# Edits to a fused attention and feed-forward kernel: prologue, last head, last tile

## The chip, the cores and the metric

The kernel runs on one core of a Trainium2 chip. The metric is the device time of one execution in microseconds. The kernel before takes 997.59 us (median of 3 runs, 997.53 to 998.23). The core has TensorE (matmul), VectorE, ScalarE and GpSimd, which run their own instruction streams and meet at semaphores, and SyncE, which issues most of the transfers.

## The reference

```python
# q, k, v: (2, 8, 768, 64), proj: (64, 6)
q_bits = (q @ proj > 0); k_bits = (k @ proj > 0)
mask = bucket(q_bits)[:, :, :, None] == bucket(k_bits)[:, :, None, :]
scores = where(mask, q @ k.T / 8, -1e9)
scores = scores - max(scores)
attn = exp(scores); attn = attn / (sum(attn) + 1e-9)
x = heads_side_by_side(attn @ v)                 # 1536 x 512
h = x @ w_in; x = (h - tanh(h)) @ w_out          # 512 -> 2048 -> 512
p = probs / (probs.sum(-1) + 1e-9)               # 4 experts
out = sum_e p[:, e] * (max(x @ w1[e], 0) @ w2[e])  # 512 -> 1024 -> 512
```

All is fp32 in and out. There are 16 heads (batch 2 by 8) of 768 tokens.

## The kernel before, in words

Matmuls are made in fp32r; where precision wants it, an operand is split into a rounded part (`hi`) and the rest (`lo`), and products of the parts are added in PSUM. The rounded parts are mostly made by ScalarE, the rests by VectorE or GpSimd.

**Attention.** Heads 0 to 15 are taken in pairs, in `pair(it)` on every engine; `b` is the head within the pair, `qt` the tile of 128 queries, `t` = 6b + qt. Per tile TensorE makes the scores (`score`, L1491, two tiles ahead of the rest), VectorE clamps them into `prob` with the row's extreme (`clamp`, L1097), ScalarE takes the exp (`take_exp`, L790), TensorE turns the six 128x128 blocks (`turn`, L1524), ScalarE rounds them out of PSUM (`round_turned`, L797) and VectorE takes the rest (`rest_turned`, L1104). From these, `weigh` (L1543) multiplies by v: the first half of a head's queries while its own tiles 4 and 5 run, the second half during tiles 1 to 3 of the next head. The results stand in `o_ps` and are moved out by ScalarE (`move_o`, L805); `weigh` waits for that move. Head 15 has no next head: its first half is moved by `move_last` and summed by VectorE (`last_sum`, L1215), its second half is made inside the first block of the feed-forward part (`finish_attention`).

**Masks.** The bits of q and k are made by four matmuls per half of the tokens (`bits`, L1480) with the projection matrix, and thresholded. They write to half of a score slot, the side slot. For head 0 the matrix has to be loaded and split first, on VectorE (L1078 to L1090).

**Inverse sums.** ScalarE's exp gives row sums; GpSimd adds eps, VectorE takes the reciprocal (`invert`, L1158), TensorE turns it (`turn_inverse`, L1489) into the side slot, VectorE copies it out (`take_inverse`, L1163), SyncE stores it to DRAM and spreads it back over 64 partitions (`spread_inverse`), and GpSimd multiplies (`x_scale`). For the last pair VectorE multiplies (`last_scale`, L1223).

**Slots.** Two PSUM slots take the scores in turn (`slot_of`). In the middle of each head one turn is left out, as the side slot is in use: the score of tile 3 goes where that of tile 2 was and waits for that tile's clamp.

**Feed-forward.** Hidden groups of 256 run in blocks of 384 tokens (`place_block`): seven products (L1596) per block by a scheme that needs sums and differences of quarters, with the down products (L1619, L1627) of the block before between them. The second part ends with six down tiles of 128 tokens by 512 columns, each added to the output by VectorE (L1299) and stored by its own DMA (L465).

The order of work on each engine is that of the code, written out by hand. A wait stands in the stream of its engine, and everything behind it on that engine waits too.

Around the change, before:

```python
for _ in range(6):                                   # TensorE, L1578: warm-up
    pe.matmul(o_ps[:, 0:HALF], x_f32[:, 0:P], x_f32[:, 0:HALF], start=True, stop=True)
...
elif qt == SIDE + first + 1 and not first:           # score: tile 4
    pe.wait_ge(inv_turn_taken, h)
```

## Time and profile before

| | |
|---|---|
| median of 3 runs | 997.59 us |
| the profiled execution | 997.7 us |
| its span, first to last instruction | 995.9 us |
| TensorE busy | 984.6 us (99%) |
| VectorE busy | 672.7 us (68%) |
| ScalarE busy | 463.3 us (47%) |
| GpSimd busy | 450.7 us (45%) |
| attention ends, first block begins | 234.20 us |

Times in the rows are microseconds from the start of the span. PE is TensorE's matmul, PEld its weight load, DVE VectorE, ACT ScalarE, POOL GpSimd, SP SyncE. L numbers are lines of the kernel before. Ends of matmuls are modelled, and a busy TensorE is not one at its peak.

### The profile page before, as it was taken

The numbers are of one execution on the slowest core, as the hardware profiler recorded it, in microseconds if no ns is written. First come the engines' busy times: TensorE is split into PE (matmuls) and PEld (weight loads), VectorE is DVE, ScalarE is ACT, GpSimd is POOL, SyncE is SP. The second block draws the span as 40 slices with busy tenths as digits, with TensorE's granted clock in tenths as the row PEclk, the third lists the DMA queues.
The fourth block names the chain that finished last, engine by engine and source line by source line (L and its number), as shares of the span: only waits on it lengthen the run. The fifth ranks groups of instructions, "written<-read, shape, count | busy, mean of one in ns | idle before, by whom it ended". The sixth has DMA issues, their size and how long they took to land.

```text
span 995.9 us, 16472 instructions
## 1 busy us (share of the span) xinstructions
PE 984.6 (99%) x5406; PEld 910.0 (91%) x5406; DVE 672.7 (68%) x1121; ACT 463.3 (47%) x853; POOL 450.7 (45%) x440
## 2 busy tenths in 40 slices
PE   7999999999999999999999999999999999999998
PEld 5999999988999999999988898989989899888997
DVE  7988888887856465565996556565565655656555
ACT  6888788887544443444542323223232232322321
POOL 6578779998664473644634304123041230412100
PEclk9999999999999999999999999999999999999999
DMA  5576656661101001010020100201002010020002
GB/s 144 160 179 178 164 161 174 170 172 36 61 22 44 22 21 63 21 42 21 22 64 22 43 22 21 63 21 42 21 21 63 21 42 21 21 64 21 21 24 102
DMA packets 50789, 65.20 MB, mean 65 GB/s; under 512 B 5345, under 2 KB 32449, under 8 KB 50753
## 3 DMA queue, kind: packets, MB, share of 16 engines
q1 hardware_dynamic: 50448, 64.48, 22.9%
q10 hardware_dynamic: 240, 0.30, 0.1%
q8 instruction: 15, 0.25, 0.1%
q14 instruction: 22, 0.17, 0.1%
q0 software_dynamic: 64, 0.00, 0.0%
HBM read 43.87 MB, written 3.19 MB: 47 GB/s over the span
## 4 chain that ended last, share of the span: by engine, by line
PE 92%; DVE 4%; POOL 1%; ACT 1%; issue 1%; DMA 0%; DVEq 0%; ACTq 0%; POOLq 0%
PE ps L1596 33%; PE ps L1619 26%; PE ps L1627 12%; PE ps L1543 7%; PE ps L1513 6%; PE ps L1524 6%; PE ps L1480 2%; DVE xq_raw L1136 1%; DVE hb L1268 1%; POOL wu_lo L622 0%; POOL g_lo L699 0%; DVE xq_lo L1148 0%; ACT wu_hi L834 0%; DVE pT_lo L1104 0%; ACT prob L790 0%
## 5 line engine op out<-in xcount | busy, mean ns | idle before, releaser
L1596 PE MATMUL ps<-xq_hi,wu_lo 128*128 128x384 f32 x672 | 227.1, 338 | 0.7 <-POOL wu_lo L622 0.4
L1596 PE MATMUL ps<-xq_hi,wu_hi 128*128 128x384 f32 x672 | 226.2, 337 | 0.0
L1596 PE MATMUL ps<-xq_lo,wu_hi 128*128 128x384 f32 x672 | 226.0, 336 | 0.0
L622 POOL TENSOR_TENSOR wu_lo<-wu_raw,wu_hi 128x768 fp32r<-128x768 f32 (+1 forms) x48 | 104.8, 2203 | 221.4 <-ACT wu_hi L834 221.3
L1299 DVE SCALAR_TENSOR_TENSOR acc<-ps,p_norm,acc 128x512 f32<-128x512 f32 x180 | 135.0, 750 | 100.9 <-PE ps L1619 95.3
L1619 PE MATMUL ps<-wd_lo,g_hi 128*128 128x512 f32 x384 | 150.9, 393 | 0.0
L1619 PE MATMUL ps<-wd_hi,g_hi 128*128 128x512 f32 x384 | 150.9, 393 | 0.0
L1619 PE MATMUL ps<-wd_hi,g_lo 128*128 128x512 f32 x384 | 150.6, 392 | 0.0
L1596 PEld LDWEIGHTS ps<-xq_hi,wu_lo 128*128 128x128 f32 x672 | 126.1, 188 | 6.6 <-DVE hb L1257 0.9
L1596 PEld LDWEIGHTS ps<-xq_lo,wu_hi 128*128 128x128 f32 x672 | 126.2, 188 | 3.8
L1596 PEld LDWEIGHTS ps<-xq_hi,wu_hi 128*128 128x128 f32 x672 | 126.1, 188 | 0.0
L989 ACT ACTIVATE g_hi<-hb 128x384 fp32r<-128x384 f32 x96 | 50.3, 525 | 161.8 <-DVE hb L1257 96.1
L699 POOL TENSOR_TENSOR g_lo<-hb,g_hi 128x384 fp32r<-128x384 f32 x64 | 72.8, 1138 | 104.5 <-ACT g_hi L912 104.5
L1104 DVE TENSOR_TENSOR pT_lo<-ps,pT_hi 128x512 fp32r<-128x512 f32 x144 | 94.7, 685 | 17.6 <-ACT pT_hi L797 17.2
L790 ACT ACTIVATE prob<-prob,neg_max 128x768 f32<-128x768 f32 x96 | 90.2, 939 | 29.2 <-DVE prob L1097 28.1
L1097 DVE TENSOR_SCALAR_CACHE_REDUCE prob<-ps 128x768 f32<-128x768 f32 x96 | 90.7, 946 | 2.9 <-PE ps L1513 2.8
L1619 PEld LDWEIGHTS ps<-wd_hi,g_hi 128*128 128x128 f32 x384 | 72.1, 188 | 16.7
L1627 PE MATMUL ps<-g_hi,wd_lo 128*128 128x384 f32 x256 | 86.1, 336 | 1.2 <-POOL g_lo L699 0.8
L1627 PE MATMUL ps<-g_hi,wd_hi 128*128 128x384 f32 x256 | 86.1, 336 | 0.0
L1627 PE MATMUL ps<-g_lo,wd_hi 128*128 128x384 f32 x256 | 85.9, 336 | 0.0
L797 ACT ACTIVATE pT_hi<-ps 128x512 fp32r<-128x512 f32 x144 | 80.3, 592 | 9.0 <-PE ps L1524 8.2
L1619 PEld LDWEIGHTS ps<-wd_hi,g_lo 128*128 128x128 f32 x384 | 72.1, 188 | 12.5
(130 smaller groups left out, 1760.7 us busy)
## 6 DMA issues: line engine op xcount, KB each, us to landing
wu_raw<-in_w SPq DMA_DIRECT2D x64, 128.0 KB, 2.8
wd_raw<-in_w SPq DMA_DIRECT2D x16, 512.0 KB, 3.3
q_raw<-in_qT SPq DMA_DIRECT2D x28, 192.0 KB, 3.2
k_raw<-in_kT SPq DMA_DIRECT2D x28, 192.0 KB, 3.3
wu_raw<-in_w_in SPq DMA_DIRECT2D x32, 128.0 KB, 2.6
wd_raw<-in_w_out SPq DMA_DIRECT2D x8, 512.0 KB, 3.5
v_raw<-in_vP SPq DMA_DIRECT2D x16, 192.0 KB, 2.8
inv_rows<-inv_dram SPq DMA_DIRECT2D x16, 192.0 KB, 3.2
```

Of the source, the lines that this page charges most:

```text
L622: rest = pool.tensor_tensor(wu[par][1][:, slots, :, :], wu_raw[:, slots, :, :], wu[par][0][:, slots, :, :].bitcast(F32), ALU.subtract)
L699: pool.tensor_tensor(g_lo[par][:, f, l * HALF:(l + 1) * HALF], hb[:, h, :], g_hi[par][:, f, l * HALF:(l + 1) * HALF].bitcast(F32), ALU.sub ...
L790: act.activation(prob[t % 3][:], prob[t % 3][:], ACT.Exp, bias=neg_max[:, t:t + 1], scale=-1.0, accum_out=total[:, t:t + 1]).then_inc(exp_ ...
L797: act.activation(pT_hi_flat[:, m * BANK:(m + 1) * BANK], turn_ps[m % 3], ACT.Copy).then_inc(pT_hi_ready, 1)
L1097: dve.tensor_scalar(prob[t % 3][:], score_ps[slot][:, 0:S], MASKED, None, ALU.min, ALU.min, accum_out=neg_max[:, t:t + 1]).then_inc(clampe ...
L1104: dve.tensor_tensor(pT_lo_flat[:, cols], turn_ps[m % 3], pT_hi_flat[:, cols].bitcast(F32), ALU.subtract).then_inc(pT_lo_ready, 1)
L1299: dve.scalar_tensor_tensor(out=part_of, in0=source, scalar=scale, in1=part_of, op0=ALU.mult, op1=ALU.add).then_inc(down_taken, 1)
L1513: mm = pe.matmul(score_ps[slot_of(b, qt, first)][:, k0:k1], x[:, rows], y[:, k0:k1], start=m == 0, stop=m == 1)
L1543: mm = pe.matmul(o_ps[:, 0:HALF].rearrange("p (t c) -> p t c", c=P), v_st[b][:, k, :], x[:, n * HT:(n + 1) * HT, k, :], start=first, stop= ...
L1596: mm = pe.matmul(to, w[:, wslot, k, :], x[:, xslot, k, :], start=start and k + m == 0, stop=k == 1 and m == 2, skip_group_check=not start)
L1619: mm = pe.matmul(to, x[:, f, rows], y[:, f, :], start=f + m == 0, stop=f == FC - 1 and m == 2)
L1627: mm = pe.matmul(to, x[:, f, rows], y[:, f, cols], start=f + m == 0, stop=f == FC - 1 and m == 2)
```

## The change

**Prologue.** The two `lo` halves of head 0's k go from GpSimd to VectorE. VectorE makes the first `lo` half of q before the projection matrix is there. The warm-up has five matmuls in place of six. **Last head.** For head 15 the score slots alternate without the turn left out; the score of tile 3 moves ahead of the weights at tile 1; the turned inverse of head 14 is no longer taken there. ScalarE's move of head 14's first half stands ahead of an exp; the move of its second half goes to VectorE. GpSimd's `x_add` stands behind `v_round` and `v_rest`. VectorE's rests of the last tile stand ahead of the reciprocal and `last_sum(0)`. **Inverses.** Those of heads 14 and 15 are turned by one transpose behind the third product of the first block and copied together; SyncE stores and spreads both. **Last tile.** The last down tile is made, added and stored as two halves of 256 columns.

```diff
-        def slot_of(b, qt, first):
-            return ((QT + 1) * b + qt + (qt >= SIDE + first)) % 2
+        def slot_of(b, qt, first, ends=False):
+            return ((QT + 1) * b + qt + (qt >= SIDE + first and not ends)) % 2
@@ SyncE
+                def spread_last():
+                    sp.wait_ge(inv_turn_taken, HEADS - 1)
+                    for b in range(2):
+                        store_inverse(HEADS - 2 + b, b)
+                    sp.wait_ge(inv_stored, 16 * HEADS)
+                    sp.wait_ge(x_ready, PAIRS - 1)
+                    for b in range(2):
+                        spread_rows(HEADS - 2 + b, b)
...
-                for k, t in enumerate(tiles_of(True)):
+                for k, t in enumerate(tiles_of(True)[:-1]):
...
+                for n in range(2):
+                    sp.wait_ge(down_taken, first_tile(I2, 0, True) + n)
+                    sp.dma_start(out[start:start + P, n * SPLIT:(n + 1) * SPLIT],
+                                 acc2[:, at + n * SPLIT:at + (n + 1) * SPLIT]).then_inc(stored, 16)
@@ GpSimd
-                            if later and b == 1:
+                            if later and b == 1 and not last:
                                 x_add(it - 1)
                         if qt == 1:
                             v_round(h, b)
                             v_rest(h, b)
+                            if last and b == 1:
+                                x_add(it - 1)
...
-                for n in range(2):
...
-                    pool.tensor_tensor(k_st[0][D:P, tokens(n)], k_raw[D:P, tokens(n)],
-                                       k_st[0][D:P, tokens(n)].bitcast(F32),
-                                       ALU.subtract).then_inc(k0_lo_ready if n == 0 else k_lo_ready, 1)
@@ ScalarE
-                        if qt == 3 and last and b == 1:
-                            move_o(h - 1, 1 - b, 1, it)
+                        if qt == 0 and last and b == 1:
+                            move_o(h - 1, 1 - b, 0, it)
                         if not (last and t == TILES - 1):
                             take_exp(i + 1, (t + 1) % TILES)
-                        if qt == 0 and not first:
+                        if qt == 0 and not first and not (last and b == 1):
@@ VectorE
+                first_q_rest(0)
                 dve.wait_ge(p_loaded, 32)
...
-                            if not first:
+                            if not first and more:
                                 take_inverse(h - 1, 1 - b, side_slot(b, first))
...
+                        if qt == 3 and last and b == 1:
+                            move_second(h - 1, 1 - b)
...
+                first_k_rest(0)
+                first_q_rest(1)
+                first_k_rest(1)
...
-                invert(HEADS - 1, 1)
...
+                rest_turned(HEADS - 1, QT - 1)
+                invert(HEADS - 1, 1)
                 last_sum(0)
-                rest_turned(HEADS - 1, QT - 1)
...
-                    if start:
-                        take_inverse(HEADS - 1, 1, slots[1])
                     first()
+                    if start:
+                        take_last_inverses()
@@ TensorE
-                    if qt == SIDE + first:
+                    if is_last(h):
+                        pe.wait_ge(clamped, i - 1)
+                    elif qt == SIDE + first:
                         pe.wait_ge(clamped, i)
...
-                        if qt != 1 + first and not (first and qt == 4):
+                        if (qt != 1 + first and not (first and qt == 4)) or not more:
                             next_score()
...
-                        if qt == 1 and not more:
-                            turn_inverse(h - 1, side_slot(b, first))
...
-                for _ in range(6):
+                for _ in range(5):
...
                 def finish_attention(part):
-                    if part == 0:
-                        turn_inverse(HEADS - 1, slots[1])
+                    if part == 1:
+                        turn_inverse(HEADS - 1, slots[0])
                     weigh(HEADS - 1, 1, 1, part)
-                    if part == 0:
-                        pe.wait_ge(inv_turn_taken, HEADS)
...
+                pe.wait_ge(inv_turn_taken, HEADS - 1)
                 place_block(0, 1, False, between=last_output)
...
+                for n in range(2):
+                    cols = slice(n * SPLIT, (n + 1) * SPLIT)
+                    pe.wait_ge(down_taken, first_tile(I2, 0, True) + n - 4)
+                    for f in range(FC):
+                        for m, (x, y) in enumerate(((h, wl), (l_, wh), (h, wh))):
+                            mm = pe.matmul(d_ps[(n + 3) % 4][:, 0:SPLIT], x[:, f, rows], y[:, f, cols],
+                                           start=f + m == 0, stop=f == FC - 1 and m == 2)
+                    mm.then_inc(down_full, 1)
```

How the change moves instructions shows in three places. The first is VectorE in the prologue, from the scalings of the projection matrix on. Before:

```order
L1078 TENSOR_SCALAR proj_f32<-proj_raw 128x6 [waits const_ready,p_loaded]
L1078 TENSOR_SCALAR proj_f32<-proj_raw 128x6 x3
L1082 CAST projq_h0<-proj_f32 64x64 [waits proj_ready]
...
L1090 TENSOR_TENSOR projq_hl<-proj_f32,projq_hl 64x64
L1190 SCALAR_TENSOR_TENSOR q_lo0<-q_raw,q_hi0 64x384 [waits q0_hi_first]
L1190 SCALAR_TENSOR_TENSOR q_lo0<-q_raw,q_hi0 64x384 [waits q_hi_ready]
L1195 TENSOR_SCALAR k_hi0<-ps,bit_from 64x384 [waits bits0_first]
```

And VectorE in the same place of the changed kernel:

```order
L1100 SCALAR_TENSOR_TENSOR q_lo0<-q_raw,q_hi0 64x384 [waits q0_hi_first]
L1114 TENSOR_SCALAR proj_f32<-proj_raw 128x6 [waits const_ready,p_loaded]
...
L1126 TENSOR_TENSOR projq_hl<-proj_f32,projq_hl 64x64
L1106 TENSOR_TENSOR k_st0<-k_raw,k_st0 64x384 [waits k0_hi_first]
L1100 SCALAR_TENSOR_TENSOR q_lo0<-q_raw,q_hi0 64x384 [waits q_hi_ready]
L1106 TENSOR_TENSOR k_st0<-k_raw,k_st0 64x384 [waits k_hi_ready]
L1236 TENSOR_SCALAR k_hi0<-ps,bit_from 64x384 [waits bits0_first]
```

One subtraction went ahead of the scalings, and two of k_st were added between the matrix and the first bits.

The second place is TensorE at tiles 0 and 1 of the last head, from the end of tile 0's turn on (prob0). Its weights for head 14 read pT and v_st0. Before:

```order
L1524 MATMUL ps<-ident,prob0 128x128
L1543 MATMUL ps<-pT_lo,v_st0 128x384 [waits o_moved,pT_lo_ready,v_lo_ready,clamped]
L1543 MATMUL ps<-pT_hi,v_st0 128x384
L1543 MATMUL ps<-pT_lo,v_st0 128x384
L1543 MATMUL ps<-pT_hi,v_st0 128x384
L1489 MATMUL ps<-ident,inverse 128x128 [waits inverted]
L1524 MATMUL ps<-ident,prob1 128x128 [waits exp_ready]
L1524 MATMUL ps<-ident,prob1 128x128
L1524 MATMUL ps<-ident,prob1 128x128 [waits pT_lo_ready]
L1524 MATMUL ps<-ident,prob1 128x128 x3
L1513 MATMUL ps<-k_hi1,q_lo1 128x512 [waits clamped]
```

And TensorE there in the changed kernel, where the four matmuls of L1569 are the score of tile 3:

```order
L1580 MATMUL ps<-ident,prob0 128x128
L1569 MATMUL ps<-k_hi1,q_lo1 128x512 [waits clamped]
L1569 MATMUL ps<-k_hi1,q_lo1 128x256
L1569 MATMUL ps<-k_st1,q_hi1 128x512
L1569 MATMUL ps<-k_st1,q_hi1 128x256
L1599 MATMUL ps<-pT_lo,v_st0 128x384 [waits pT_lo_ready,o_moved,v_lo_ready]
L1599 MATMUL ps<-pT_hi,v_st0 128x384
L1599 MATMUL ps<-pT_lo,v_st0 128x384
L1599 MATMUL ps<-pT_hi,v_st0 128x384
L1580 MATMUL ps<-ident,prob1 128x128 [waits exp_ready]
```

The score stands ahead of the weights, and the turn of the inverse is gone.

The third place is VectorE from the last head's last clamp (prob2) into the first block. Before:

```order
L1097 TENSOR_SCALAR prob2,neg_max<-ps 128x768 [waits score_full]
L1104 TENSOR_TENSOR pT_lo<-ps,pT_hi 128x512 [waits pT_hi_ready] x3
L1158 RECIPROCAL inverse<-total_eps 128x6 [waits eps_added]
L1215 TENSOR_TENSOR x_f32<-ps,pv_other 64x384 [waits x_ready,o_moved]
L1104 TENSOR_TENSOR pT_lo<-ps,pT_hi 128x512 [waits pT_hi_ready] x2
L1163 COPY inv_turned<-ps 6x128 [waits inv_turn_full]
L1247 TENSOR_TENSOR hb<-ps,hb 128x384 [waits c1_ready,sum11_full]
L1268 TENSOR_TENSOR hb<-hb,tanh_h0 128x384 [waits tanh_ready]
```

And VectorE there in the changed kernel, with the added move of o_ps (pv0) as the first row:

```order
L1204 COPY pv0<-ps 128x384 [waits o_full]
L1133 TENSOR_SCALAR prob2,neg_max<-ps 128x768 [waits score_full]
L1140 TENSOR_TENSOR pT_lo<-ps,pT_hi 128x512 [waits pT_hi_ready] x5
L1194 RECIPROCAL inverse<-total_eps 128x6 [waits eps_added]
L1255 TENSOR_TENSOR x_f32<-ps,pv_other 64x384 [waits x_ready,o_moved]
L1293 TENSOR_TENSOR hb<-ps,hb 128x384 [waits c1_ready,sum11_full]
L1272 COPY inv_turned<-ps 38x128 [waits inv_turn_full]
L1314 TENSOR_TENSOR hb<-hb,tanh_h0 128x384 [waits tanh_ready]
```

The sum over o_ps (x_f32) moved behind the last two rests of pT, and the copy of the inverses behind the block's first sum.

## Rows read from the trace of the kernel before

**Rows 1.** Page, section 1: busy us (share of the span) xinstructions

```profile
PE 984.6 (99%) x5406; PEld 910.0 (91%) x5406; DVE 672.7 (68%) x1121; ACT 463.3 (47%) x853; POOL 450.7 (45%) x440
```

**Rows 2.** Busy time by stretch: us; PE, PEld, DVE, ACT, POOL; PEclk, DMA, GB/s

```profile
0.00:24.00 24.00, 18.98 (x88) 13.98 (x89) 18.30 (x46) 15.38 (x29) 14.67 (x28) 1.00 0.55 142
...
248.30:985.00 736.70, 735.67 (x3844) 685.62 (x3845) 454.46 (x695) 261.57 (x454) 251.98 (x203) 1.00 0.11 35
```

**Rows 3.** Timeline, prologue: start, us, engine, line, operation [idle before <-releaser]

```profile
5.57 1.00 POOL L676 TENSOR_TENSOR k_st<-k_raw,k_st 64x384 fp32r<-64x384 f32 x1 [1.88 <-ACT k_st L773]
5.65 0.97 DVE L1082 CAST projq_h<-proj_f 64x64 fp32r<-64x64 f32 x1
...
6.86 0.22 DVE L1086 TENSOR_TENSOR projk_ll<-proj_f,projk_hh 128x64 fp32r<-128x64 f32 x1
...
7.01 1.00 POOL L676 TENSOR_TENSOR k_st<-k_raw,k_st 64x384 fp32r<-64x384 f32 x1 [0.44 <-ACT k_st L773]
7.09 0.99 DVE L1088 TENSOR_TENSOR projq_h<-proj_f,projk_hh 64x64 fp32r<-64x64 f32 x1
...
8.26 1.02 DVE L1190 SCALAR_TENSOR_TENSOR q_lo<-q_raw,q_hi 64x384 fp32r<-64x384 f32 x2
...
9.07 0.41 PE L1480 MATMUL ps<-q_lo,projq_h 128*128 128x384 f32 x1 [1.36 <-DVE q_lo L1190]
```

**Rows 4.** Timeline, ScalarE in the prologue

```profile
3.94 0.53 ACT L770 ACTIVATE q_hi<-q_raw 64x384 fp32r<-64x384 f32 x1
```

**Rows 5.** Timeline, TensorE's weight loads in the warm-up

```profile
5.35 0.34 PEld L1579 LDWEIGHTS ps<-x_f 128*128 128x128 f32 x1 [0.30 <-issue]
...
5.94 1.16 PEld L1579 LDWEIGHTS ps<-x_f 128*128 128x128 f32 x4 [0.25 <-issue]
```

**Rows 6.** Timeline, last head

```profile
222.93 0.49 ACT L805 ACTIVATE pv<-ps 128x384 f32<-128x384 f32 x1
...
223.67 0.41 PE L1543 MATMUL ps<-pT_lo,v_st 128*128 128x384 f32 x1 [0.82 <-ACT pv L805]
...
224.96 0.67 DVE L1104 TENSOR_TENSOR pT_lo<-ps,pT_hi 128x512 fp32r<-128x512 f32 x1
...
229.67 0.95 DVE L1097 TENSOR_SCALAR_CACHE_REDUCE prob<-ps 128x768 f32<-128x768 f32 x1
...
232.29 0.44 PE L1524 MATMUL ps<-ident,prob 128*128 128x128 f32 x2 [0.36 <-DVE pT_lo L1104]
```

**Rows 7.** Chain of work that ended last, one score: start us, us, what

```profile
216.55 0.70 PE ps L1513 x4
```

**Rows 8.** Timeline, end of the last head and first block; page, section 6

```profile
234.20 0.42 PE L1596 MATMUL ps<-xq_hi,wu_lo 128*128 128x384 f32 x1
...
234.34 0.56 DVE L1215 TENSOR_TENSOR x_f<-ps,pv_other 64x384 f32<-64x384 f32 x1
...
234.96 1.29 DVE L1104 TENSOR_TENSOR pT_lo<-ps,pT_hi 128x512 fp32r<-128x512 f32 x2
...
236.40 0.42 PE L1543 MATMUL ps<-pT_lo,v_st 128*128 128x384 f32 x1
...
247.17 1.82 DVE L1223 TENSOR_TENSOR acc<-x_f,inv_rows 128x384 f32<-128x384 f32 x2
...
248.25 0.41 PE L1627 MATMUL ps<-g_hi,wd_lo 128*128 128x384 f32 x1 [0.83 <-POOL g_lo L699]
...
inv_rows<-inv_dram SPq DMA_DIRECT2D x16, 192.0 KB, 3.2
```

**Rows 9.** The end: chain, timeline, and busy time of one stretch

```profile
984.46 8.22 PE ps L1619 x36
...
992.70 0.75 DVE L1299 SCALAR_TENSOR_TENSOR acc<-ps,p_norm,acc 128x512 f32<-128x512 f32 x1 [0.61 <-PE ps L1619]
993.47 0.33 SPq L465 DMA_DIRECT2D out<-acc  x1
...
994.25:995.05 0.80, 0.00 (x0) 0.00 (x0) 0.00 (x0) 0.00 (x0) 0.00 (x0) 1.00 0.87 328
```

More of the change, by code:

```diff
@@ L1074, in _, with first_q_rest, first_k_rest @@
                 dve.memset(projq_h0[D:P, qs].bitcast(F32), 0.0)
+                def first_q_rest(n):
+                    dve.wait_ge(q0_hi_first if n == 0 else q_hi_ready, 1)
+                    dve.scalar_tensor_tensor(out=q_lo[0][0:D, tokens(n)], in0=q_raw[0:D, tokens(n)], scalar=QSCALE,
+                                             in1=q_hi[0][0:D, tokens(n)].bitcast(F32), op0=ALU.mult,
+                                             op1=ALU.subtract).then_inc(q0_lo_first if n == 0 else q_lo_ready, 1)
+                def first_k_rest(n):
+                    dve.wait_ge(k0_hi_first if n == 0 else k_hi_ready, 1)
+                    dve.tensor_tensor(k_st[0][D:P, tokens(n)], k_raw[D:P, tokens(n)],
+                                      k_st[0][D:P, tokens(n)].bitcast(F32),
+                                      ALU.subtract).then_inc(k0_lo_ready if n == 0 else k_lo_ready, 1)
+                first_q_rest(0)
                 dve.wait_ge(p_loaded, 32)
@@ L1171, in pair @@
                             ahead = (t + 1) % TILES
-                            clamp(i + 1, ahead, slot_of(ahead // QT, ahead % QT, first and qt < QT - 1))
+                            clamp(i + 1, ahead, slot_of(ahead // QT, ahead % QT, first and qt < QT - 1,
+                                                        is_last(2 * it + ahead // QT) and t < TILES - 1))
                         if first and qt == 2:
@@ L1185, in pair @@
                             invert(h - 1, 1 - b)
-                for n in range(2):
-                    dve.wait_ge(q0_hi_first if n == 0 else q_hi_ready, 1)
-                    dve.scalar_tensor_tensor(out=q_lo[0][0:D, tokens(n)], in0=q_raw[0:D, tokens(n)], scalar=QSCALE,
-                                             in1=q_hi[0][0:D, tokens(n)].bitcast(F32), op0=ALU.mult,
-                                             op1=ALU.subtract).then_inc(q0_lo_first if n == 0 else q_lo_ready, 1)
+                        if qt == 3 and last and b == 1:
[3 more added lines that the diff above has]
+                first_k_rest(1)
                 def first_bits(n, to, own, done):
@@ L1512, in score @@
                         for k0, k1 in ((0, BANK), (BANK, S)):
-                            mm = pe.matmul(score_ps[slot_of(b, qt, first)][:, k0:k1], x[:, rows], y[:, k0:k1],
+                            mm = pe.matmul(score_ps[slot_of(b, qt, first, is_last(h))][:, k0:k1], x[:, rows], y[:, k0:k1],
                                            start=m == 0, stop=m == 1)
@@ L1711, in _ @@
                         place_block(i, r, True)
-                for k in range(BT):
+                for k in range(BT - 1):
                     down_tile(I2 - 1, 3, True, k)
+                (wh, wl), h, l_ = wd[1], g_hi[1], g_lo[1]
+                rows = slice(tiles_of(True)[BT - 1] * P, (tiles_of(True)[BT - 1] + 1) * P)
+                for n in range(2):
+                    cols = slice(n * SPLIT, (n + 1) * SPLIT)
[5 more added lines that the diff above has]
+                    mm.then_inc(down_full, 1)
 def kernel(**inputs):
```

55 lines of the change are left out of this document (38 added, 17 removed).

## The prediction

> **What bounds the kernel now.** I read the busy shares first: TensorE is busy 984.6 of the span's 995.9 us [rows 1]. Then the stretches: from 248.3 to 985 us TensorE is busy 735.67 of 736.70 us, in the first 24 only 18.98 [rows 2]. So nothing off TensorE's path counts in the long middle, and whatever time a start gains there is carried to the end undiminished. The change lives where TensorE waits: the prologue, the last head with the first block behind it, and the tail after the last matmul. The timeline of each says what it waits for. The profiled execution took 997.7 us, 1.8 more than its span; the median of the runs is 997.59, so I make the sum against 997.7 and take 0.1 off. What a measurement can tell from no change is 0.2%, 2.0 us: faster means below 995.6.
>
> **Prologue.** The first projection matmul starts at 9.07, when VectorE has run a chain that began with the projection matrix's arrival and ends with q_lo [rows 3]. Two links stand out. A cast of 64x64 starts at 5.65 and takes 0.97 us; a subtraction of 64x64 starts at 7.09 and takes 0.99. A subtraction of 128x64, with GpSimd quiet, takes 0.22. GpSimd's two k_st subtractions run at 5.57 to 6.57 and 7.01 to 8.01, and the slow VectorE instructions end 0.05 and 0.07 after them. The change takes these two off GpSimd. If the long durations are the wait for GpSimd, 0.97-0.22 = 0.75 and 0.99-0.22 = 0.77, 1.52 together, go; if they belong to the 64x64 forms themselves, nothing goes. No row has such a form with GpSimd quiet, so the bounds are 0 and 1.6; I take 1.5, since both ends fit GpSimd's.
> The Trainium skill (SBUF — State Buffer, Who interferes with whom) says the pair of ports that VectorE shares with GpSimd is locked for a whole instruction, and that casts and instructions with two SBUF inputs can be held. By it the gain is the full 1.5; with long forms as the cause it would be 0. The trace agrees in both ends.
>
> What VectorE gets in return: the first q_lo half goes ahead of the matrix (ScalarE's q_hi starts at 3.94 and takes 0.53 [rows 4]; 0.51 long by the pair's 1.02, it is over by 5.0, and the cast's own inputs, four small scalings of the matrix, are made right before 5.65), so it costs nothing. In its old place stands one k_st half of the same size, again about 0.5 (between 0.5, the pair's half, and GpSimd's 1.00). The first group of four matmuls thus starts at about 9.07-1.5 = 7.55. The second group now needs a q_lo half and a k_st half more: VectorE ends them 1.0 after the first, about 8.3, and TensorE would reach them four matmuls (of 0.175 each: twelve such take 2.1 in the first block [rows 8]) after 7.55, at 8.25. At most 0.2 is lost, and VectorE's own next work, the first bits, waits only for the first group. ScalarE's part is not touched and runs ahead of its readers. GpSimd's later steps (the scaling of head 1) wait for ScalarE, not for the removed work, so they stay where they are; their cover is the first scores and exps that TensorE has to get through before head 1's bits. Warm-up: one matmul of six goes, 0.58 us at the quick pace; six end at some 7.4 and would just stand in front of a start at 7.5. Term: **-1.5**, bounds 0 and -1.6.
>
> The warm-up's weight load at 5.35 takes 0.34 after 0.30 of idleness, 0.64 in all; from 5.94 four come in 1.16 us [rows 5]. TensorE then rests until 9.07 and still works at the quick pace. In the changed kernel it works 0.6 us less and rests less. The granted clock of the stretch is 1.00, the 2.4 GHz level [rows 2]. I see no reason for a slow start, and keep it as a rival.
> The Trainium skill (TensorE: Matmul & The Clock Gate, What's actually happening) says that the clock rises by TensorE having been busy and falls by idleness. It speaks against a shorter warm-up; by it the start could be slow, which is rival 4. The trace has the quick pace before the last four loads, two of which stay.
>
> **Last head.** Before, TensorE stands 0.82 us until 223.67, waiting for ScalarE's move of o_ps that starts at 222.93; VectorE's first rest of head 15 stands until 224.96 behind the copy of the turned inverse, though its input is there at 223.9 [rows 6]. (Times between the rows shown are read from the same timeline.) Now score 9 needs an older clamp (slots alternate), stands ahead of the weights, and fills that hole: it costs the 0.70 that four score matmuls take [rows 7] but runs at 222.7 to 223.4; the move stands before an exp and is done at 222.5. The weights then go at 223.4 and the turn at 224.1 (224.55 before). VectorE rests tile 6 at 223.95 and clamps tile 9 at 224.6. Not all of that lasts: ScalarE's row of exp, round, x_round is full until 225.6 in both kernels, so the rests of tile 7 end at 227.5. Clamp 10 follows at 227.5, a rest at 228.4, then the added move on VectorE (0.56 like the 64x384 sum of rows 8), which puts clamp 11 at 229.65, where it was (229.67). What improves is behind it: ScalarE, rid of a move (0.49 in rows 6) and with its exp 10 from 228.4, rounds tile 9 by 230.4 instead of 231.9, so VectorE's rests start at 230.55 instead of 231.55. TensorE starts head 15's weights at 229.75 (230.21) and the second part of turn 10, which waited for VectorE until 232.29, at 231.25. From there on the work is the same, and the first block, at 234.20 before [rows 8], starts near 233.15: **-1.05**. Bounds: 0, if the added move makes VectorE the bound, and -1.5, the 1.0 of that rest and the move's 0.49.
>
> Queued behind what is moved: on GpSimd, x_add now comes after v_round and v_rest, which had waited behind it for a DMA; they come earlier and x_add no later. On SyncE, the two inverse rows of head 14 go to the end with those of head 15. Both are issued at about 238, spread at 241 and have landed at 244 (3.2 us each); their reader, last_scale, starts at 247.17, less some 0.6 [rows 8]. It is covered by 2 us and more; were it not, last_scale would hold VectorE and with it the second block.
>
> **First block.** Here the change costs. Before, the sum over o_ps runs at 234.34, in the hole before the last rests, which run from 234.96 to 236.25; weights start at 236.40, when TensorE's first twelve products end [rows 8]. Now the sum and a reciprocal (0.1) stand behind the rests, and the weights wait for the sum: 236.25+0.1+0.56 = 236.9, plus 0.05, against 236.4. That is 0.55 to 0.65 later, measured from the block's start. The inverse's turn leaves this place for one behind the third product, 0.1 each way. The copy of both inverses holds VectorE in order until that turn, so the first tanh subtraction starts some 0.7 later, but its reader on TensorE comes 8 us on. A part is given back: TensorE waited 0.83 us at 248.25 for GpSimd's g_lo, a chain that starts with ScalarE and GpSimd steps which keep their early time; the wait for it shrinks by 0.1 to 0.5. Net of the block: **+0.45**, bounds +0.1 and +0.7.
>
> **End.** The last tile takes six matmuls of 512 columns; VectorE's 0.75 at 992.70 follows; the store's issue at 993.47; its data move in one burst from 994.25 to 995.05 [rows 9]. Halved: twelve of 256 columns. Scores hold two of 512 and two of 256 in 0.70 [rows 7], the wide ones 0.228 apart (36 in 8.22 us), so a narrow one costs 0.12, and twelve cost 1.44 against 1.37: +0.07. VectorE's last instruction is half as wide: between 0.38 (half) and 0.56 (384 columns); I take 0.40, -0.35. The last store carries half the bytes: its burst is 0.35 shorter at the same rate; rows of 1 KB instead of 2 may eat a part, and the first half's burst may queue behind the tile before. I take -0.2, bounds 0 and -0.35. Term: **-0.5**, bounds -0.2 and -0.65.
>
> **Sum.** -1.5-1.05+0.45-0.5 = -2.6; 997.7-2.6 = 995.1, and 0.1 off for the median: **995.0**.
>
> **Rivals.**
> 1. The last head gives nothing: VectorE, with a move more, bounds it, and the late sum eats the rest. For it: clamp 11 comes no earlier in my walk. Against: ScalarE is rid of the same work. -1.5-0.5, 995.6; or 995.8 with a loss of 0.2.
> 2. The prologue gives little: the 64x64 forms are long by themselves, or a k_st half on VectorE takes 1.0. For it: no row of the form alone. Against: both ends match. -0.3-0.6-0.5 = -1.4, 996.2.
> 3. All ends well: the rests come early enough for the late sum to be hidden, and the stall at 248.25 takes up the block's loss: -1.6-1.4-0.6, some 994.0.
> 4. Slower: TensorE's clock is at 1.2 GHz when the bits start, for want of the sixth warm-up matmul. The place is 7.5 us; it decides if the quick pace has not come or is lost by then. Of the 18.98 us that TensorE is busy in the first 24, some 11 lie behind that point, and would double until it rises; two thirds of that on the path is +7, so -2.6+7: 1002. Against it: the quick pace came at 5.94 [rows 5], before the last four loads.
>
> **How the numbers follow.** Forecast 0.57 (own range 994.5 to 995.5), rival 1 0.16, rival 2 0.13, rival 3 0.10, rival 4 0.04. Faster by over 0.2%: 0.54 of the forecast, 0.10 of rival 3, half of rival 1, none of rival 2: 0.71. Slower: rival 4, 0.04, and 0.01 for the rest. Same: 0.24. The range of 8 in 10 reaches from rival 3 to rival 2: 993.9 to 996.3.
>
> **What would show it.** In the profile of the changed kernel: the 64x64 cast and subtraction near 0.2 us and the first projection matmul near 7.5; no wait for ScalarE's move at the last head's second tile; the first block's first matmul 2.5 us earlier than 234.20; a wait of about 0.6 on the sum over o_ps ahead of the weights in it; last_scale not waiting for a DMA; a last VectorE instruction near 0.4. The prediction is wrong if the cast stays at 1 us, if TensorE's steps at 8 us are twice as long, or if the block starts less than 2 us earlier.

## The result and the profile after

The changed kernel takes **994.51 us** (median of 7 runs, 994.20 to 994.84) against 997.59 (7 runs); the ratio is 0.9967, 95% interval [0.9955, 0.9978]. The profiled execution has a span of 992.7 us against 995.9. So 3.2 us are gone in the profile, 3.1 in the medians; 2.6 were forecast. The busy shares of the page barely move:

```profile
PE 984.2 (99%) x5409; PEld 909.9 (92%) x5409; DVE 672.5 (68%) x1124; ACT 462.4 (47%) x852; POOL 447.9 (45%) x438
```

By stretch (columns as in [rows 2]), the first 24 us hold 1.36 us more of TensorE's work than before, and the stretch from 248.30 on holds the same 735.67:

```profile
0.00:24.00 24.00, 20.34 (x98) 15.30 (x99) 19.20 (x51) 16.25 (x30) 14.51 (x27) 1.00 0.58 149
...
248.30:985.00 736.70, 735.67 (x3841) 685.18 (x3840) 454.95 (x693) 258.93 (x450) 251.52 (x203) 1.00 0.11 34
```

The prologue's timeline, which answers to [rows 3]:

```profile
4.48 0.55 DVE L1100 SCALAR_TENSOR_TENSOR q_lo<-q_raw,q_hi 64x384 fp32r<-64x384 f32 x1 [1.36 <-ACT q_hi L792]
...
5.00 0.39 DVE L1114 TENSOR_SCALAR proj_f<-proj_raw 128x6 f32<-128x6 f32 x4
...
5.42 0.19 DVE L1118 CAST projq_h<-proj_f 64x64 fp32r<-64x64 f32 x1
...
6.08 0.22 DVE L1124 TENSOR_TENSOR projq_h<-proj_f,projk_hh 64x64 fp32r<-64x64 f32 x1
...
6.36 0.56 DVE L1106 TENSOR_TENSOR k_st<-k_raw,k_st 64x384 fp32r<-64x384 f32 x1
...
7.06 0.41 PE L1534 MATMUL ps<-q_lo,projq_h 128*128 128x384 f32 x1 [0.16 <-DVE k_st L1106]
...
8.23 0.41 PE L1534 MATMUL ps<-q_lo,projq_h 128*128 128x384 f32 x1 [0.23 <-DVE k_st L1106]
```

The cast fell from 0.97 to 0.19, the subtraction from 0.99 to 0.22. The second group waits 0.23 for a k_st half. The first bits matmul moved from 9.07 to 7.06. 0.23 of that is a scaling of the projection matrix that begins earlier in this execution (at 5.00, at 5.23 in the kernel before): the matrix landed at most 2.9 us after its issue instead of 3.2, and the scalings stand right behind the query half, without a wait.

The last head and the first block, which answer to [rows 6] and [rows 8]:

```profile
231.32 0.42 PE L1650 MATMUL ps<-xq_hi,wu_lo 128*128 128x384 f32 x1
...
233.50 0.56 DVE L1255 TENSOR_TENSOR x_f<-ps,pv_other 64x384 f32<-64x384 f32 x1
...
234.16 0.41 PE L1599 MATMUL ps<-pT_lo,v_st 128*128 128x384 f32 x1 [0.51 <-DVE x_f L1255]
...
245.49 0.41 PE L1681 MATMUL ps<-g_hi,wd_lo 128*128 128x384 f32 x1 [0.21 <-POOL g_lo L721]
```

The block begins at 231.32 instead of 234.20. The weights wait 0.51 for the late sum, as foreseen, but the wait for g_lo shrinks from 0.83 to 0.21 and gives most of the loss back. VectorE's `last_scale` starts without a wait for a DMA, as foreseen too. The end, by the chain of work that ended last and the timeline ([rows 9]):

```profile
988.57 1.44 PE ps L1774 x12
...
990.04 0.48 DVE L1509 SCALAR_TENSOR_TENSOR acc<-ps,p_norm,acc 128x256 f32<-128x256 f32 x1 [0.23 <-PE ps L1774]
```

**Where the 3.2 us lie.** I cut the path at four marks that both kernels have: the first score, ScalarE's first round of the last head, the first matmul of the block, the matmul that waits for g_lo. The changed kernel was profiled a second time (label after_again below), with VectorE's first scaling of the projection matrix at 5.23 as before; that profile is the fair one to subtract. The scaling stands at 5.23 for another reason there: the matrix has landed (3.0 us after its issue, 3.2 in the kernel before), but the query half ahead of it runs from 4.75, as ScalarE's rounding of it came at 4.20 and not at 3.93. The first two marks in the timeline of the kernel before:

```profile
12.02 0.61 PE L1513 MATMUL ps<-k_hi,q_lo 128*128 128x512 f32 x2 [1.29 <-DVE k_hi L1195]
...
221.03 1.09 ACT L797 ACTIVATE pT_hi<-ps 128x512 fp32r<-128x512 f32 x2 [0.39 <-PE ps L1524]
```

and in the changed kernel's second profile:

```profile
10.30 0.61 PE L1569 MATMUL ps<-k_hi,q_lo 128*128 128x512 f32 x2 [0.90 <-DVE k_hi L1236]
...
219.42 1.09 ACT L819 ACTIVATE pT_hi<-ps 128x512 fp32r<-128x512 f32 x2 [0.36 <-PE ps L1580]
```

| stretch | before | changed, second profile | difference |
|---|---|---|---|
| start to first score | 12.02 | 10.30 | -1.72 |
| to the last head's first round | 209.01 | 209.12 | +0.11 |
| to the block's first matmul | 13.17 | 11.90 | -1.27 |
| to the matmul waiting for g_lo | 14.05 | 14.17 | +0.12 |
| to the span's end | 747.65 | 747.21 | -0.44 |

The second row lies between 208.8 and 209.7 over all the profiles, with the same instructions. Two places make most of its scatter. A bits matmul near 68 us stands for a transfer in score_back and whole_tile, and a score near 61.7 us comes late by 0.15 to 0.49 in eight of the thirteen profiles of the other kernels, in both of the changed kernel among them. In order, score_back, then the first and the second profile of the changed kernel, whose rows name no releaser, then probe_write, whose row names one:

```profile
68.72 0.44 PE L1534 MATMUL ps<-q_lo,projq_h 128*128 128x384 f32 x1 [0.34 <-DMA q_lo<-k_st]
61.62 0.30 PEld L1569 LDWEIGHTS ps<-k_hi,q_lo 128*128 128x128 f32 x2 [0.34 <-issue]
61.70 0.30 PEld L1569 LDWEIGHTS ps<-k_hi,q_lo 128*128 128x128 f32 x2 [0.21 <-issue]
62.51 0.61 PE L1576 MATMUL ps<-k_hi,q_lo 128*128 128x512 f32 x2 [0.26 <-DMA k_hi<-bits_kq]
```

The one profile of the kernel before has no such gap. So the +0.11 may be the landing of a transfer that differs from run to run, or a piece of the prologue's gain that is lost because TensorE now reaches this place earlier; one profile of the kernel before doesn't decide it. VectorE's first scaling also starts anywhere from 4.96 to 5.36. So below I read a small effect from the stretch in which the edit lies, and give the median beside it.

### The profile page after: what moved, and what is told of

Same layout as the page of the kernel before. It is cut to its first block, busy times and chain, and to the rows that moved or that the text cites. A ratio compares the mean times of both kernels' runs of the same rounds, so it can differ in the third digit from the quotient of the medians.

```text
span 992.7 us, 16478 instructions
## 1 busy us (share of the span) xinstructions
PE 984.2 (99%) x5409; PEld 909.9 (92%) x5409; DVE 672.5 (68%) x1124; ACT 462.4 (47%) x852; POOL 447.9 (45%) x438
## 4 chain that ended last, share of the span: by engine, by line
PE 92%; DVE 4%; ACT 1%; POOL 1%; issue 1%; DMA 0%; DVEq 0%; ACTq 0%; POOLq 0%
PE ps L1650 33%; PE ps L1673 26%; PE ps L1681 12%; PE ps L1599 7%; PE ps L1569 6%; PE ps L1580 6%; PE ps L1534 2%; DVE xq_raw L1172 1%; DVE hb L1314 1%; POOL wu_lo L651 0%; DVE pT_lo L1140 0%; POOL g_lo L721 0%; DVE xq_lo L1184 0%; ACT wu_hi L856 0%; ACT pT_hi L819 0%
```

## The experiments

All were run in three sets, each with the kernel before on the same chip (997.63 to 997.68). The changed kernel itself is in the third set only (994.28, where the first set of its runs gave 994.51), so a difference of 0.2 between medians of different sets says nothing.

**k_on_pool.** The key rests back on GpSimd; the early query half stays on VectorE.

```diff
-                first_k_rest(0)
-                first_k_rest(1)
+                pool.tensor_tensor(k_st[0][D:P, tokens(n)], k_raw[D:P, tokens(n)],
+                                   k_st[0][D:P, tokens(n)].bitcast(F32), ALU.subtract)
```

> The changed kernel with one part of the prologue undone: the two halves of the key rest (64x384) are again worked out by GpSimd; the early first query half on VectorE stays. Theory (what the prologue gained is that GpSimd no longer runs an operation with two SBUF inputs beside VectorE's 64x64 casts): the two casts go from 0.19 and 0.22 back to 0.97 and 0.99 us, the first bits matmul comes 1.0 to 1.6 us later than 7.06, and the kernel takes 995.5 to 996.0 against 994.5. Rival (the casts are quick because the query half was put ahead of them, or because 64x64 costs what it costs on a given day): casts stay near 0.2 us, first matmul within 0.2 of 7.06, time 994.5.

Measured: 995.44 (994.99 to 995.99), ratio 0.9978 [0.9969, 0.9987]. Timeline of its prologue:

```profile
5.71 1.00 POOL L707 TENSOR_TENSOR k_st<-k_raw,k_st 64x384 fp32r<-64x384 f32 x1 [2.02 <-ACT k_st L804]
5.79 0.96 DVE L1127 CAST projq_h<-proj_f 64x64 fp32r<-64x64 f32 x1
...
7.14 0.99 POOL L707 TENSOR_TENSOR k_st<-k_raw,k_st 64x384 fp32r<-64x384 f32 x1 [0.44 <-ACT k_st L804]
7.22 0.99 DVE L1133 TENSOR_TENSOR projq_h<-proj_f,projk_hh 64x64 fp32r<-64x64 f32 x1
```

The long forms are back at once, and the first bits matmul is 1.35 later (8.41); the time is just under the range expected. From the matrix's scaling to the first score it takes 6.02 us; the changed kernel takes 5.07, the kernel before 6.79. So of the prologue's 1.72 the key rests on VectorE are worth 0.95 once the query half is ahead, and the query half put ahead is worth 0.77. This is the swap that the prediction counted: the query half leaves the path, a key half of 0.56 takes its place, and the two instructions that GpSimd held give back 1.55.

**probe_read.** Nothing is undone; work that nobody reads is added on GpSimd.

```diff
+                pool.memset(acc[:, 6, :], 0.0)
+                # when the key halves are rounded, n = 0, 1:
+                pool.tensor_tensor(acc[D:P, 6, tokens(n)], acc[D:P, 6, tokens(n)], acc[D:P, 6, tokens(n)], ALU.add)
```

> The changed kernel with work added on GpSimd alone that nothing waits for: a clearing of a spare tile and, at the two moments at which the kernel before worked out the key rests, two additions of that tile to itself (64x384, two SBUF inputs). VectorE keeps all that the change gave it. Theory of the held port: though no data hangs on them, they bring the casts of 64x64 back to near 1 us, hold the rests on VectorE too, and put the first bits matmul 1.0 to 1.7 us later: 995.5 to 996.2. Rival (order on VectorE did it, GpSimd's work only mattered by its results): nothing moves, 994.5.

Measured: 995.86 (995.44 to 996.19), ratio 0.9983 [0.9974, 0.9992], 1.35 over the changed kernel's first median. Its timeline:

```profile
5.51 0.19 DVE L1125 CAST projq_h<-proj_f 64x64 fp32r<-64x64 f32 x1
5.58 0.82 POOL L707 TENSOR_TENSOR acc<-acc 64x384 f32<-64x384 f32 x1 [1.22 <-ACT k_st L802]
5.62 0.84 DVE L1126 CAST projk_hh<-proj_f 128x64 fp32r<-128x64 f32 x1
...
7.02 0.86 POOL L707 TENSOR_TENSOR acc<-acc 64x384 f32<-64x384 f32 x1 [0.61 <-ACT k_st L802]
...
7.11 1.19 DVE L1113 TENSOR_TENSOR k_st<-k_raw,k_st 64x384 fp32r<-64x384 f32 x1
```

The 64x64 cast, begun before GpSimd's addition, keeps its 0.19; the next one, of 128x64, is held until that addition ends (6.46 against 6.40). The subtraction of 64x384 is held too, 1.19 instead of 0.56, and ends 0.42 after the second addition. Shape is not the point; who is running is. The result of these additions is read by nobody, so GpSimd's running alone does it. This settles rival 2 of the prediction against it.

**probe_write.** The same two moments, with two clearings instead of two additions.

```diff
-                    pool.tensor_tensor(acc[D:P, 6, tokens(n)], acc[D:P, 6, tokens(n)], acc[D:P, 6, tokens(n)], ALU.add)
+                    pool.memset(acc[:, 6, :], 0.0)
```

> As the earlier run with two added GpSimd additions, but with two clearings (128x768, 0.73 us each) in their place, at the same moments. If any work of GpSimd on SBUF holds VectorE, the casts or rests beside it take 0.7 us longer and the first score comes 0.5 to 1.4 us later: 995.0 to 995.9. If only an operation that reads two SBUF operands does, nothing is held: 994.5 within 0.2.

Measured: 994.82 (994.35 to 995.40), ratio 0.9970 [0.9959, 0.9981]. The first score is at 10.89 against 10.30. Neither expectation holds whole:

```profile
5.25 0.94 DVE L1121 TENSOR_SCALAR proj_f<-proj_raw 128x6 f32<-128x6 f32 x4
5.39 0.77 POOL L707 MEMSET acc<- 128x768 f32 x1 [1.02 <-ACT k_st L802]
...
6.84 0.74 POOL L707 MEMSET acc<- 128x768 f32 x1 [0.68 <-ACT k_st L802]
6.90 0.22 DVE L1131 TENSOR_TENSOR projq_h<-proj_f,projk_hh 64x64 fp32r<-64x64 f32 x1
...
7.18 0.55 DVE L1113 TENSOR_TENSOR k_st<-k_raw,k_st 64x384 fp32r<-64x384 f32 x1
```

The first of these two clearings holds the four small scalings (0.94 instead of 0.37 to 0.39, their end 0.03 after its end); the second runs across three subtractions with two SBUF inputs and holds none (0.22 and 0.55, as with GpSimd quiet). The Trainium skill (SBUF — State Buffer, Who interferes with whom) draws this very line: an instruction with two SBUF inputs collides with GpSimd's reads and not with its writes, while casts and tensor-scalar forms can take the whole shared pair and collide with either. The rows agree for the subtractions and for the tensor-scalar form; a cast beside a clearing didn't come up here.

**warm0.** No warm-up matmul.

```diff
-                for _ in range(5):
+                for _ in range(0):
```

> The changed kernel without any of its five warm-up matmuls. If TensorE's clock is granted from the first real matmul on anyway, nothing moves (994.5, first quick pitch at once). If the clock stands at 1.2 GHz until TensorE has worked for a while, the bits, first scores and turns run at twice their time until it rises; the window from 7 to 12 us holds some 3 us of busy TensorE, so up to 2 to 3 us are lost there: 996 to 997.5. That prices the rival in which one warm-up fewer costs the clock.

Measured: 996.13, with times in two groups: 994.84 to 994.91 (3 runs) and 995.93 to 996.56 (8). The profile is of one in the first group (994.84). Its first bits matmuls are 0.32 us apart, where they are 0.17 apart with the warm-up, though the granted clock reads 1.00:

```profile
7.71 0.52 PE L1534 MATMUL ps<-q_hi,projq_hl 128*128 128x384 f32 x1
8.03 0.52 PE L1534 MATMUL ps<-k_st,projk_ll 128*128 128x384 f32 x1
...
11.34 0.51 PE L1569 MATMUL ps<-k_st,q_hi 128*128 128x512 f32 x2
```

By the first scores the pace is the quick one again. In this profile it costs 0.60 from the scaling to the first score (5.67 against 5.07). What the other eight runs lose beyond that, about 1.4 more (their median is 996.3), no profile shows; it stays open. The price of a slow start is thus some 0.6 to 2 us here, not the 7 of rival 4, and with five warm-ups it isn't paid at all: the bits matmuls of both profiles of the changed kernel are 0.17 apart.

**no_last_head.** Prologue and end as changed, last head and block as before (the two groups of edits taken into the kernel before).

> The kernel before with the prologue edits (early query half, key rests on VectorE, five warm-ups) and the halved last tile, but with the last head and the first block as they were. Theory by the traces: the prologue's -1.6 and the end's -0.5 stay, the last head's -1.27 and the block's +0.12 are gone, so +1.15 against the changed kernel: 995.6 (995.2 to 996.0). Rival (the prologue's gain is swallowed by the last head's wait for the spread rows if the head is left as it was): 996.5 or more.

Measured: 995.58 (995.25 to 996.28), ratio 0.9980 [0.9971, 0.9989]; expected 995.6. From the last head's first round to the g_lo matmul it takes 27.21 us, against 27.22 in the kernel before and 26.07 in the changed one: the last head and block are worth 1.14. It has the old waits, all of them:

```profile
221.60 0.41 PE L1561 MATMUL ps<-pT_lo,v_st 128*128 128x384 f32 x1 [0.82 <-ACT pv L804]
222.68 0.28 DVE L1175 COPY inv_turned<-ps 6x128 f32<-6x128 f32 x1 [0.86 <-PE ps L1507]
224.04 0.96 DVE L1109 TENSOR_SCALAR_CACHE_REDUCE prob<-ps 128x768 f32<-128x768 f32 x1 [0.48 <-PE ps L1531]
...
230.22 0.44 PE L1542 MATMUL ps<-ident,prob 128*128 128x128 f32 x2 [0.36 <-DVE pT_lo L1116]
```

**Three single undos in the last head.** move1_back puts the first move behind the exponential again, act_move the second move back on ScalarE, score_back the score of the second tile behind the weights and the turn.

```diff
move1_back
-                        if qt == 0 and last and b == 1:
-                            move_o(h - 1, 1 - b, 0, it)      # ahead of take_exp
-                        if qt == 0 and not first and not (last and b == 1):
+                        if qt == 0 and not first:            # behind take_exp
act_move
-                            move_second(h - 1, 1 - b)        # VectorE
+                            move_o(h - 1, 1 - b, 1, it)      # ScalarE
score_back
-                        if (qt != 1 + first and not (first and qt == 4)) or not more:
+                        if qt != 1 + first and not (first and qt == 4):
```

> The changed kernel with the first move of the last head behind the exponential on ScalarE again, as in the other heads. Theory A (the 0.82 us wait of the kernel before at the last head's first weights is that of this order alone): the first weights of the last head wait 0.6 to 0.8 us for pv, 0.5 to 0.8 us are lost: 995.0 to 995.3. Theory B (with the score issued a tile earlier, ScalarE's two operations stand before TensorE needs the bank, and the order is worth nothing): 994.5 within 0.15.

> The changed kernel with the second move of the last pair's values back on ScalarE, at its old place, instead of on VectorE. Theory A (ScalarE is the one that TensorE waits for in the last head, so 0.55 us more on it come back as waits for its rounds and exponentials): +0.3 to +0.6, 994.8 to 995.1. Theory B (the head was freed by the early first move and by the slots that alternate; the second move has slack on either engine): within 0.15 of 994.5.

> The changed kernel with the score that the last head issues at its second tile behind the weights and the turn again, as in the other heads; the score slots still alternate and nothing else is changed. Theory A (the score moved up is what keeps VectorE and ScalarE fed in the last head): TensorE waits 0.3 to 0.7 us more for the turned probabilities, 994.8 to 995.2. Theory B (only the order of equal work on TensorE, which has no wait there either way): within 0.15 of 994.5.

| | median | first round of the last head to g_lo matmul | against the changed kernel's 26.07 |
|---|---|---|---|
| move1_back | 994.41 | 26.10 | +0.03 |
| act_move | 995.05 | 26.56 | +0.49 |
| score_back | 994.61 | 26.18 | +0.11 |

move1_back has no wait for pv at all, and score_back lies within its theory B. act_move has the wait that theory A names; its chain starts at ScalarE, whose second move waits 0.78 for TensorE and pushes the next round:

```profile
226.85 0.49 ACT L827 ACTIVATE pv<-ps 128x384 f32<-128x384 f32 x1 [0.78 <-PE ps L1599]
...
228.16 1.07 ACT L819 ACTIVATE pT_hi<-ps 128x512 fp32r<-128x512 f32 x2
...
229.53 0.44 PE L1580 MATMUL ps<-ident,prob 128*128 128x128 f32 x2 [0.36 <-DVE pT_lo L1142]
```

score_back has a wait of 0.25 at its second tile, of which 0.11 is left later. The three sum to 0.63 of the 1.15 by which this stretch is shorter than before. The rest lies in what none of them undoes (the alternating slots, the inverse's turn and copy taken out of the head, GpSimd's and VectorE's new order), or in edits that cover for one another: move1_back may be worth nothing only because the score now stands ahead of the weights. Neither was tried, so how the last head's gain divides is in part open.

**sum_first and shift_halves.** Two attempts at a kernel that beats the changed one: the block's late sum put into VectorE's idle 1.02 us before 232.09; and on top of it the last pair's values shifted across the partitions in two halves.

```diff
+                last_sum(0)
                 rest_turned(HEADS - 1, QT - 1)
                 invert(HEADS - 1, 1)
-                last_sum(0)
```

```diff
-                            shift_part(h - 1, 1 - b, it)     # 2 transfers of 192 KB after the second move
+                            shift_halves(h - 1, it)          # 2 of 96 KB after each move
```

> The changed kernel with one thing moved on VectorE after the last head: the sum of the block's first half (x_f, 0.56 us) is put ahead of the last tile's rest and of the inverse of the last head, where VectorE idles 1.02 us before 232.09. Theory (the 0.51 us wait of TensorE at 234.16 for that sum is real and nothing later takes it up): the wait goes, the last weights come about 0.1 to 0.4 us sooner or, where the rest that is now behind the sum is late in its turn, nothing is gained: 994.1 to 994.4. Rival (the sum needs rows that land only at about 232, so VectorE now stands still before the rest and the weights for the rest come later than before): 994.6 to 995.2.

> The kernel with the sum put first (sum_first) and one thing more: the last pair's values are shifted across the partitions in two halves, each sent when its own half is moved, so that only half of the bytes leave at 227.9. In sum_first TensorE's wait at 234.16 is gone, but the one for g_lo at 245.5 grew from 0.21 to 0.74, and before it GpSimd works without a pause from 231.5, where it had waited 1.41 us for this transfer. Theory (GpSimd's chain from that landing sets the wait for g_lo): the landing is 0.4 to 0.7 earlier, the g_lo wait falls to 0.1 to 0.3, and the time is 0.3 to 0.6 under the changed kernel's: 993.9 to 994.3. Rival (the landing is by latency and not by bytes, or VectorE and the last sums hold the block): 994.5 as sum_first.

Measured: 994.58 (994.25 to 995.12) and 994.34 (994.11 to 995.03): no difference from 994.51 and 994.28, and less than either theory wanted. From the last head's first round to the g_lo matmul they take 25.97 and 25.95 against 26.07, 0.1 less. In sum_first the wait of 0.51 is gone, the block runs 0.5 ahead, and nearly all of it is waited away at one place, from 0.21 to 0.74:

```profile
231.54 0.56 DVE L1255 TENSOR_TENSOR x_f<-ps,pv_other 64x384 f32<-64x384 f32 x1 [0.41 <-ACT pv_other L834]
...
239.89 1.01 POOL L721 TENSOR_TENSOR g_lo<-hb,g_hi 128x384 fp32r<-128x384 f32 x1
240.09 1.23 DVE L1314 TENSOR_TENSOR hb<-hb,tanh_h 128x384 f32<-128x384 f32 x1
...
241.95 3.36 POOL L721 TENSOR_TENSOR g_lo<-hb,g_hi 128x384 fp32r<-128x384 f32 x2 [1.05 <-ACT g_hi L934]
...
242.41 2.04 DVE L1189 TENSOR_TENSOR wd_lo<-wd_raw,wd_hi 128x1024 fp32r<-128x1024 f32 x1
...
245.46 0.41 PE L1681 MATMUL ps<-g_hi,wd_lo 128*128 128x384 f32 x1 [0.74 <-POOL g_lo L721]
```

The hb subtraction has two SBUF inputs; it starts earlier than in the changed kernel (there 240.63, 0.61 us) and so falls longer under GpSimd's g_lo, and takes 1.23. It ends 0.42 after that g_lo, as the held 64x384 subtraction of probe_read did, and within 0.1 of its end in the changed kernel (241.24). In shift_halves the landing is 0.87 earlier (GpSimd starts at 230.65 instead of 231.52), more than I had expected, yet the wait for g_lo stays at 0.75 instead of falling, because GpSimd then waits for ScalarE:

```profile
230.65 1.82 POOL L590 TENSOR_TENSOR x_f<-x_f,pv_other 64x768 f32<-64x768 f32 x1 [0.60 <-DMA pv_other<-pv]
...
233.43 1.85 POOL L629 TENSOR_TENSOR xq_lo<-xq_raw,xq_hi 128x768 fp32r<-128x768 f32 x1 [0.95 <-ACT xq_hi L863]
235.33 4.53 POOL L662 TENSOR_TENSOR wu_lo<-wu_raw,wu_hi 128x768 fp32r<-128x768 f32 x2
239.81 1.00 POOL L732 TENSOR_TENSOR g_lo<-hb,g_hi 128x384 fp32r<-128x384 f32 x1
```

So the block is set by this row: ScalarE's rounding of x, then GpSimd's 1.85, 4.53 and 1.00 without a pause; behind it VectorE's held subtraction, two more of its instructions, and wd_lo, 2.04 long, beside which GpSimd's last g_lo runs. That g_lo ends 0.86 to 0.88 after wd_lo in these two profiles, in no_last_head, in the kernel before and in the changed one, and the matmul follows. Neither edit touches the start of the row. From the block's first matmul to the g_lo matmul it takes 14.05 in the kernel before and in no_last_head and 14.06 and 14.05 here, whatever TensorE waited on the way; the changed kernel takes 14.17, and that 0.1 is all that its wait of 0.51 costs.

**whole_tile.** The last tile whole: six matmuls of 512 columns and one store, for twelve of 256 and two (TensorE's part is shown).

```diff
-                for k in range(BT - 1):
+                for k in range(BT):
                     down_tile(I2 - 1, 3, True, k)
-                (wh, wl), h, l_ = wd[1], g_hi[1], g_lo[1]
...
```

> The changed kernel with the last tile of 128x512 whole again: one pass of six long matmuls instead of twelve of 256 columns, one VectorE operation (0.75 us) and one output transfer. Theory: the halved tile hides half of the last sum and of the transfer's start behind TensorE; without it the end is later by 0.47 us: 994.9 to 995.1. Rival (the transfer's own latency, about 2 us whatever its size, sets the end, and halving moved only the records): within 0.15 of 994.5.

Measured: 995.08 (994.46 to 995.25), ratio 0.9971 [0.9960, 0.9982]. From the g_lo matmul to the span's end it takes 747.73 us against 747.21: 0.52, by the last tile alone, as the theory has it; the rival doesn't hold.

**after_again.** The changed kernel once more.

> The changed kernel, unaltered, so that its profile and time stand beside the other runs of this set. Expected 994.5 (994.2 to 994.9). The profile of the changed kernel has one wait of about 0.35 us at 61 us that the kernel before has not, and two of the variants show one of 0.24 and 0.34 near 68 us for the transfer q_lo<-k_st. If such waits belong to the change, this profile has one too, in the same place; if they are chance in the landing of a transfer, it has none or one elsewhere.

Measured: 994.28 (994.11 to 994.49). Its middle is 0.23 shorter than in the first profile, its first scaling 0.23 later; the block starts at 231.32 in both. It has the gap at 61.7 too, 0.21 instead of 0.34, in the same place. By what I had written down this speaks for a wait that belongs to the change; against it stand five profiles that have none (act_move, no_last_head, probe_read, warm0, whole_tile), three of them with the first score as early (10.26, 10.03, 10.31). It isn't settled. The wait near 68 us is in two profiles and not in these.

## Why the prediction was right, and where its steps were off

The forecast was 995.0 with 994.5 to 995.5 as its own range; 994.51 lies at its lower edge, and the 994.28 of after_again below it. All four places gave or cost with the sign foreseen, but three of the four terms were too cautious, so the errors add up instead of cancelling.

- **Prologue, -1.5 foreseen, -1.72 measured.** The mechanism (VectorE held by GpSimd) is shown by k_on_pool and probe_read. The bound of -1.6 was too tight. From the cast's start to that of the half ahead of the bits it took 2.61 us (5.65 to 8.26 [rows 3]) and takes 0.94 (5.42 to 6.36): 1.67 instead of the 1.52 that I had from the two durations alone. The cast and the subtraction give 0.78 each, and the pause ahead of the half is 0.11 shorter; the handover from VectorE to TensorE takes 0.14 where it took 0.26. First matmul foreseen at 7.55, found at 7.06, in the second profile at 7.28. That the query half ahead of the matrix "costs nothing" doesn't hold whole: in both profiles the scalings stand right behind it, in the second some 0.2 us after the matrix landed (an estimate, from 5.23 and the 3.0 us that it took from an issue near 2.0). Nor does the middle pass a gain on undiminished for certain: 0.11 is missing behind it, in a place where the kernel before loses nothing.
- **Last head, -1.05 foreseen, -1.27 measured.** The size is near, the reason given was in part another. I gave the early first move on ScalarE a part ("the move stands before an exp"); move1_back shows that, with the other edits in place, it is worth nothing. My own walk had said so: left behind the exp it ends at 222.93 + 0.49 = 223.42, and I had the weights go at 223.4. The step that held is the one on ScalarE rid of the second move, 0.49 by act_move. I also had VectorE's clamp 11 unmoved at 229.65; it starts at 227.75, 0.3 earlier than the shift of the whole head by 1.61 would have it, and the rests behind it follow 0.3 earlier, which is the 0.22 that the term lacked. Up to clamp 10 the walk holds within 0.1; from there I had added whole durations (0.9, 0.69, 0.56), while the instructions start 0.87, 0.60 and 0.47 apart (225.81, 226.68, 227.28, 227.75).
- **First block, +0.45 foreseen, +0.12 measured.** The term that was mis-sized: the loss was as worked out, the weights 0.64 later from the block's start (2.84 against 2.20; 0.55 to 0.65 foreseen), and 0.75 by the last product (13.63 against 12.88). But 0.63 of it came back at the wait for g_lo, where I had taken 0.15 and allowed 0.5 at most. sum_first shows why: that wait is set by the row from ScalarE's last rounding of x, which keeps its place whatever TensorE does before it. A delay ahead of such a wait is free up to about the wait's length.
- **End, -0.5 foreseen, -0.44 to -0.52 measured.** VectorE's half took 0.48, not 0.40, which gives 0.27 and not 0.35; the narrow matmuls are 0.12 apart as worked out; the bytes of the last store made up the difference: the data move is over at about 991.8, 1.3 us after VectorE, where it took 1.6 before, so 0.3 and not 0.2.

Of the rivals, 1 (the last head gives nothing) and 2 are refuted by no_last_head and probe_read. Rival 3 named the block's recovery rightly, and the result lies midway between it (994.0) and the forecast. Rival 4 didn't happen, and by warm0 its price was set at least three times too high: it let the slow pace last to 24 us, and in the one profile it was over by 10.9.

## What to carry to other kernels

Before an instruction on VectorE is called slow by its shape, look at what GpSimd runs at that moment. The mark is an end soon after GpSimd's end, by 0.03 to 0.1 us for the small forms here and by 0.42 for subtractions of 384 columns. Moving GpSimd's work onto VectorE (two halves, 1.00 us each there, 0.56 here) can then make VectorE's own row shorter. Where a stall stands before a wait on another engine's row, removing it gives little (0.1 of 0.5 us here), and adding one costs little; find the row that sets the last wait (here ScalarE's rounding, three GpSimd operations and what hangs on them) before touching what lies ahead of it. An undo of each edit alone is worth its run: one that I had argued for did nothing while the others stood.

## What the runs showed of the hardware that I had not expected

- A clearing on GpSimd, which reads nothing, holds VectorE's tensor-scalar forms (0.94 against 0.37 us for four) and leaves its two-input subtractions alone (0.22 and 0.55 us).
- Without warm-up the bits matmuls ran at 0.32 us apart instead of 0.17 while the granted clock of the profile read 1.00, which is the level of 2.4 GHz. A spacing nearly twice as long is what the level of 1.2 GHz would give; here the spacing showed the slow start and the column didn't.
- Shifting values across the partitions in halves of 96 KB, the first sent early, instead of 192 KB at once (two such transfers) brought the start of the work that waits for them 0.87 us forward, for two issues more on SyncE. From issue to landing the halves take 2.0 and 2.2 us, the whole transfers 3.0 and 3.4 in the changed kernel (medians of the page's section 6).
